# Later attention carried between the products of the layers

## The chip, the cores and the metric

One core of one Trainium2 chip runs the whole program. The metric is the device time of one execution in microseconds. The kernel before took 971.6 us (median of 3 runs, 970.73 to 973.06).

## What is computed

Three stages in a row, all in 32-bit floats:

```python
scores = scale * q @ k.T                    # 4 batches, 8 heads, 576 tokens, head width 64
scores = where(0 <= i - j < 128, scores - slope[h] * |i - j|, -1e9)
x = softmax(scores) @ v                     # then heads side by side: 2304 tokens x 512
x = (sigmoid(x @ w_gate) * (x @ w_val)) @ w_out      # hidden width 1536
out = ((x @ w1) * (x @ w2)) @ w3 @ w_out2            # hidden width 1024
```

## The kernel before

**Precision.** Each 32-bit operand is split into a high part (rounded to TensorE's fast 32-bit form) and a low part, the rest. A product is three matmuls: high x high, high x low, low x high (`product`, lines 424 to 426). The high part is a copy on ACT (sometimes DVE), the low part a subtraction on POOL or DVE.

**Attention.** A pair of heads of one batch is 5 steps of up to 128 queries, so 16 pairs are 80 steps. Step n passes through slots: scores (slot n + 4), masked and negated scores with their minimum on DVE (n + 5), exponentials on ACT, the row sums plus 1e-9 and their reciprocal on DVE, normalising on POOL (n + 6), four transposes on TensorE (n + 7), high and low part of the transposes, value product (n + 9), copy into `xf`. The queries of two heads stand as a block diagonal, so a scores matmul uses all 128 rows; a step is two blocks of 64 queries against 192 keys each. The program also multiplies `w3 @ w_out2` once (the fold): 64 products of 512 columns, one a slot, stored to memory. Attention has its own eight PSUM banks, laid under those of the layers.

**Layers.** The 2304 tokens go in three passes of 768, each in two halves of 384. A layer works in groups of 256 hidden columns (6 in the first, 4 in the second, where w3 is already in the folded output weights). Per group, `x @ w_gate` and `x @ w_val` (or w1, w2) are each a 2 x 2 block product done with seven block products and extra additions (`multiply`, `combine`); each block product is 6 matmuls of 384 columns. Sums of x (five tiles of its blocks, once per layer and pass) and sums of weights (once per group, on POOL in `weight_sum`) go in. Three banks hold the products, two the gates, three the output projection (`project`), which adds 8 tiles per group into `xf` (`add_up`). The projection of a group runs after the next group's products; the last one of a layer follows directly. Each engine's order is written out by hand, and engines meet by semaphores. Weights of group g + 1 are split while group g is multiplied (`weights_hi_plain`, `weights_hi_sums`, `weights_lo`). Where a layer begins, POOL also makes parts of the new x.

## Time and profile before

| | |
|---|---|
| profiled execution | 972.31 us, span 970.5 us |
| runs | 970.73, 971.6, 973.06 us |
| busy share | TensorE 93%, its weight loads 90%, DVE 71%, ACT 52%, POOL 74% |
| granted TensorE clock, mean | 0.979 |
| chain that ended last | TensorE 71%, DVE 14%, ACT 7%, issue 5%, POOL 2% |

The page shows one execution on the hardware profiler. PE is TensorE's matmuls, PEld its weight loads, SP the queue that issues the DMAs. A matmul's duration is its way through a pipeline: the next starts long before it ends, so throughput is read from starts. Idle time counts only on the engine that sets the end.

### The profile page before, as it was taken

To read this page: it belongs to the slowest core of one execution; us is meant where nothing else is said; L and a number is where in the kernel's file an instruction comes from. 1 tells how busy PE (TensorE), PEld (TensorE's weight loads), DVE (VectorE), ACT (ScalarE), POOL (GpSimd) and SP (SyncE) were. 2 spreads that over 40 slices of the span, in tenths; PEclk is the share of its full clock that TensorE was granted. 3 is DMA by queue.
4 is the path that set the end of the run, shared out by engine and by line. 5 is a ranking of instruction groups with operands and counts; after the bars stand their busy time and mean duration, and the time that the engine had idled before them with its cause. 6 is when DMAs were issued, how large, how long until landed. Compare 5 with 4: busy or idle time off the path is not lost.

```text
span 970.5 us, 15723 instructions
## 1 busy us (share of the span) xinstructions
PE 899.5 (93%) x5272; PEld 869.0 (90%) x5272; DVE 689.1 (71%) x1506; ACT 505.8 (52%) x1139; POOL 722.3 (74%) x535
## 2 busy tenths in 40 slices
PE   3999989868999997999999999799999999989998
PEld 3889877767899997899889999789988999988998
DVE  7988899885666668577756666857785666686666
ACT  4888878767544443544454444354444444435441
POOL 6778877876887775998679777489867977738940
PEclk9999999979999999999999999999999999998999
DMA  7333432410222210222142222012113211211301
GB/s 235 105 108 113 121 95 78 143 47 23 86 76 78 66 66 22 72 82 69 41 140 79 66 83 71 22 66 87 66 44 131 87 66 66 67 42 52 102 1 66
DMA packets 37409, 75.92 MB, mean 78 GB/s; under 512 B 3153, under 2 KB 16081, under 8 KB 37329
## 3 DMA queue, kind: packets, MB, share of 16 engines
q1 hardware_dynamic: 37328, 74.92, 23.9%
q8 instruction: 42, 0.69, 0.3%
q14 instruction: 39, 0.31, 0.1%
HBM read 68.09 MB, written 6.82 MB: 77 GB/s over the span
## 4 chain that ended last, share of the span: by engine, by line
PE 71%; DVE 14%; ACT 7%; issue 5%; POOL 2%; DMA 1%; SPq 0%; ACTq 0%; DVEq 0%; POOLq 0%
PE quad_ps L424 15%; PE quad_ps L426 14%; PE quad_ps L425 14%; PE o_ps L424 8%; PE o_ps L426 8%; PE o_ps L425 8%; DVE rowsum L766 3%; DVE xs_lo L811 2%; ACT exps L584 2%; DVE negs L755 1%; DVE xf L879 1%; POOL prob L1007 1%; ACT pt_hi L595 1%; DVE pt_lo L775 1%; ACT wq_hi L630 1%
## 5 line engine op out<-in xcount | busy, mean ns | idle before, releaser
L424 PE MATMUL quad_ps<-xs_hi,wq_hi 128*128 128x384 f32 x840 | 286.9, 342 | 25.4 <-ACT s L646 22.0
L426 PE MATMUL quad_ps<-xs_hi,wq_lo 128*128 128x384 f32 x840 | 284.6, 339 | 0.0
L425 PE MATMUL quad_ps<-xs_lo,wq_hi 128*128 128x384 f32 x840 | 284.5, 339 | 0.0
L424 PEld LDWEIGHTS quad_ps<-xs_hi,wq_hi 128*128 128x128 f32 x840 | 160.8, 191 | 31.7 <-issue 16.5
L1041 POOL TENSOR_TENSOR wq_lo<-wsum,wq_hi 128x1280 fp32r<-128x1280 f32 x60 | 177.3, 2955 | 9.4 <-ACT wq_hi L630 9.4
L424 PE MATMUL o_ps<-h_hi,wo_hi 128*128 128x384 f32 x480 | 161.2, 336 | 3.2 <-DVE xf L879 3.1
L425 PEld LDWEIGHTS quad_ps<-xs_lo,wq_hi 128*128 128x128 f32 x840 | 160.7, 191 | 0.0
L426 PEld LDWEIGHTS quad_ps<-xs_hi,wq_lo 128*128 128x128 f32 x840 | 160.5, 191 | 0.0
L426 PE MATMUL o_ps<-h_hi,wo_lo 128*128 128x384 f32 x480 | 160.4, 334 | 0.0
L425 PE MATMUL o_ps<-h_lo,wo_hi 128*128 128x384 f32 x480 | 160.4, 334 | 0.0
L1037 POOL TENSOR_TENSOR wq_lo<-raw_q,wq_hi 128x512 fp32r<-128x512 f32 x60 | 77.7, 1295 | 105.8 <-ACT wq_hi L624 105.8
L879 DVE TENSOR_TENSOR xf<-o_ps,xf 128x384 f32<-128x384 f32 x192 | 103.5, 551 | 43.6 <-PE o_ps L426 43.6
L661 ACT ACTIVATE gate_ps<-side 128x384 f32<-128x384 f32 x120 | 59.6, 498 | 76.4 <-DVE h_lo L867 55.4
L424 PEld LDWEIGHTS o_ps<-h_hi,wo_hi 128*128 128x128 f32 x480 | 90.1, 188 | 5.8 <-DVE xf L879 5.8
L646 ACT COPY s<-quad_ps 128x384 f32<-128x384 f32 x60 | 28.7, 479 | 120.2 <-PE quad_ps L426 120.1
L425 PEld LDWEIGHTS o_ps<-h_lo,wo_hi 128*128 128x128 f32 x480 | 90.1, 188 | 0.0
L426 PEld LDWEIGHTS o_ps<-h_hi,wo_lo 128*128 128x128 f32 x480 | 90.1, 188 | 0.0
L668 ACT CAST h_hi<-gate_ps 128x384 fp32r<-128x384 f32 x120 | 57.6, 480 | 59.6 <-DVE gate_ps L862 59.6
L1047 POOL TENSOR_TENSOR wo_lo<-raw_o,wo_hi 128x1024 fp32r<-128x1024 f32 x30 | 72.0, 2401 | 17.9 <-ACT wo_hi L638 17.9
L584 ACT ACTIVATE exps<-negs,negmax 128x192 f32<-128x192 f32 (+1 forms) x144 | 62.0, 432 | 42.9 <-DVE negmax L755 40.9
L867 DVE TENSOR_TENSOR h_lo<-gate_ps,h_hi 128x384 fp32r<-128x384 f32 x120 | 65.9, 549 | 23.8 <-ACT h_hi L668 23.3
L1062 POOL TENSOR_TENSOR wsum<-raw_q 128x512 f32<-128x512 f32 x60 | 81.8, 1363 | 0.0
(89 smaller groups left out, 1893.8 us busy)
## 6 DMA issues: line engine op xcount, KB each, us to landing
raw_q<-w SPq DMA_DIRECT2D x24, 512.0 KB, 3.5
raw_q<-w_gate SPq DMA_DIRECT2D x18, 512.0 KB, 3.5
raw_q<-w_val SPq DMA_DIRECT2D x18, 512.0 KB, 3.5
raw_o<-w_out SPq DMA_DIRECT2D x18, 512.0 KB, 3.5
raw_o<-w_times_wout SPq DMA_DIRECT2D x12, 512.0 KB, 3.6
k_raw<-kT SPq DMA_DIRECT2D x16, 288.0 KB, 2.9
q_raw<-qT SPq DMA_DIRECT2D x16, 288.0 KB, 3.0
v_raw<-v SPq DMA_DIRECT2D x16, 256.0 KB, 2.7
```

Source lines behind the costliest of these rows:

```text
L424: pe.matmul(out, lh, rh, start=start, stop=False, skip_group_check=onto)
L425: pe.matmul(out, lh, rl, start=False, stop=False, skip_group_check=onto)
L426: return pe.matmul(out, ll, rh, start=False, stop=stop, skip_group_check=onto)
L584: op = nc.scalar.activation(exps[buf][:, cols], negs[buf][:, cols], ACT.Exp, scale=-1.0, bias=negmax[:, 2 * buf + j:2 * buf + j + 1], accu ...
L661: nc.scalar.activation(gate_ps[n % 2][:, 0:TH], side[:, piece(k)], func).then_inc(gated, 1)
L668: nc.scalar.copy(h_hi[g % 2][:, piece(k)], gate_ps[n % 2][:, 0:TH]).then_inc(h_hi_done, 1)
L867: nc.vector.tensor_tensor(out=h_lo[g % 2][:, piece(k)], in0=gate_ps[n % 2][:, 0:TH], in1=h_hi[g % 2][:, piece(k)], op=ALU.subtract).then_i ...
L879: op = nc.vector.tensor_tensor(out=xf[:, cols], in0=ps_o[t % 3][:, 0:TH], in1=xf[:, cols], op=ALU.add)
L1037: nc.gpsimd.tensor_tensor(out=wq_lo[m][:, cols].rearrange("p (b n) -> p b n", b=2), in0=four[:, 0:4:3, :], in1=wq_hi[m][:, cols].rearrange ...
L1041: nc.gpsimd.tensor_tensor(out=wq_lo[m][:, 0:5 * GW], in0=wsum[m][:, :], in1=wq_hi[m][:, 0:5 * GW], op=ALU.subtract).then_inc(wq_split[m], 1)
L1047: nc.gpsimd.tensor_tensor(out=wo_lo[g % 2][:, :], in0=raw_o[:, :], in1=wo_hi[g % 2][:, :], op=ALU.subtract).then_inc(wo_split, 1)
L1062: op = nc.gpsimd.tensor_tensor(out=out[:, 2 * GW:4 * GW], in0=raw[:, 0:2 * GW], in1=raw[:, 2 * GW:4 * GW], op=ALU.subtract)
```

## The change

- **Attention is cut by thirds of the tokens.** The 80 steps are ordered by pass. The 28 of the first third (`HEAD`) run ahead of the layers, with two folds a slot. The other 52 are carried one per section inside the layers of pass one (24) and pass two (28).
- **Sections.** The layers' work is now a list of sections: gate (seven products), value (seven products), projection (eight tiles). A section issues the scores of step n first. The step of the section before has its transposes after the third product (or the third tile) and its value product after the sixth (or the seventh tile).
- **A step** is 128 queries of each of two heads against up to 256 keys. The scores are matmuls on 64 rows, heads alternating, each in its own bank. Softmax works in place in one tile. The addition of 1e-9 moves from DVE to ACT.
- **The block product** uses another formula with seven products and four sums of weights; products 1 and 2, and 7 and 4, accumulate in one bank. Results stay in four banks and the gate is kept in SBUF; no gate bank. The projection has two banks, attention two.
- **Tiles.** `xf` holds two thirds. Loaded raw tiles lie under the low parts that they become; the first loads wait for DVE's memsets. POOL makes four weight sums, a low part of three plain blocks and a low part of four sums.
- **x parts.** Of a layer's seven x blocks three are plain and four are sums; POOL makes one sum and four low parts (P1, P7, P3, P4), DVE the rest.

```diff
+PARTS = (((0, 0, 3), (0, 384, 2), (1, 0, 2)), ((1, 192, 3), (2, 0, 3)), ((2, 384, 2), (3, 0, 3), (3, 384, 2)))
+JOBS = [(third, hp, b, q0, n) for third in range(NPASS) for hp in range(HP) for b, q0, n in PARTS[third]]
+STEP = [(j, i) for j, job in enumerate(JOBS) for i in range(job[4])]
+FIRST = [STEP.index((j, 0)) for j in range(len(JOBS))]
...
+STEPS_TO = [sum(n for third, _, _, _, n in JOBS if third < t) for t in range(NPASS + 1)]
...
+P1, P5, P6, P2, P7, P3, P4 = range(7)
...
+A21, A11, A12, A22 = range(4)
...
+HALF_OF = {0: (C11, C12), 1: (C21, C22)}
+BANK_OF = {P1: 0, P2: 0, P6: 1, P3: 1, P5: 2, P7: 3, P4: 3}
+BANK_OUT = {C11: 0, C12: 1, C22: 2, C21: 3}
...
+LAG_QK, LAG_SCORE, LAG_NORM, LAG_TURN, LAG_PV = 3, 4, 5, 6, 8
+SLOTS = HEAD + LAG_PV
...
+def fold_slot(k):
+    return 5 + k // 2
+FOLDS_IN = [[k for k in range(NFOLD - IB) if fold_slot(k) == s] for s in range(SLOTS)]
...
+SECTIONS = []
+for g_ in range(NG):
+    SECTIONS += [(g_, "gate", g_), (g_, "val", g_)]
+    if not first_of(g_):
+        SECTIONS.append((g_, "proj", g_ - 1))
+    if last_of(g_):
+        SECTIONS.append((g_, "proj", g_))
...
+def step_at(sec):
+    t = sec // PASS_SECTIONS + 1
+    n = STEPS_TO[t] + sec % PASS_SECTIONS if sec >= 0 and t < NPASS else NSTEP
+    return n if t < NPASS and n < STEPS_TO[t + 1] else None
...
+        def twin(scope, name, shape):
+            with ExitStack() as first:
+                loaded = sb(first, f"{name}_raw", shape, F32)
+            return loaded, sb(scope, name, shape, F32R)
...
+        quad = [ps(f"quad_ps{k}") for k in range(4)]
+        ps_o = [ps(f"o_ps{k}") for k in range(2)]
+        attn = [ps(f"attn_ps{k}") for k in range(2)]
...
+            sp.wait_ge(zeroed, 1)
...
+                wait(pe, scored, n)
+                if n >= HEAD:
+                    drained = n in STEPS_TO
+                    pe.wait_ge(pt_split, n if drained else n - 1)
+                    pe.wait_ge(x_ready, n if drained else n - 1)
+                keys, q = keys_of(n), slice(i * P, (i + 1) * P)
+                first = JOBS[j][3] + (i - 1) * P - key_base(j)
+                where = slice(first + keys.start, first + keys.stop)
+                sides = ((q_hi, k_hi), (q_hi, k_lo), (q_lo, k_hi))
+                for t, (left, right) in enumerate(sides):
+                    for h in range(2):
+                        rows = slice(h * D, (h + 1) * D)
+                        mm = pe.matmul(score_bank(n, h)[:, keys], left[st][rows, q], right[st][rows, where],
+                                       start=t == 0, stop=t == 2)
                 mm.then_inc(qk_done, 1)
...
+            def consumed(q, blk):
+                if q % 2:
+                    pe.wait_ge(gated, 4 * (q // 2) + blk + 1)
+                else:
+                    wait(pe, h_split, 4 * (q // 2 - 1) + blk + 1)
...
+                if first_of(g) and m == 0:
+                    pe.wait_ge(xs_split[j], instance(g) + 1)
+                if j == P1:
+                    if q == 0:
+                        pe.wait_ge(scored, HEAD)
+                    else:
+                        consumed(q, C11)
+                elif j == P5:
+                    if q == 0:
+                        pe.wait_ge(pt_split, HEAD)
+                    else:
+                        consumed(q, C22)
+                elif j == P6 and q > 0:
+                    consumed(q, C12)
+                elif j == P7 and q > 0:
+                    consumed(q, C21)
+                elif j == P2:
+                    pe.wait_ge(s1_done, q + 1)
+                elif j == P3:
+                    pe.wait_ge(u2_done, q + 1)
+                elif j == P4:
+                    pe.wait_ge(c_done[C22], q + 1)
...
+                pe.wait_ge(h_split, 4 * g + 1 + max(HALF_OF[0][c], HALF_OF[1][c]))
+                wait(pe, acc_done, t - 1)
...
+            for k in range(NFOLD - IB, NFOLD):
+                fold(k)
+            for sec, (g, kind, of) in enumerate(SECTIONS):
+                n, m = step_at(sec), step_at(sec - 1)
+                if n is not None:
+                    scores(n)
+                if kind == "proj":
+                    for k in range(8):
+                        project(of, k)
+                        if k == 2 and m is not None:
+                            turn(m)
+                        if k == 6 and m is not None:
+                            pv(m)
                 else:
+                    for j in range(7):
+                        multiply(2 * g + (kind == "val"), j)
+                        if j == P6 and m is not None:
+                            turn(m)
+                        if j == P3 and m is not None:
+                            pv(m)
...
+                act.wait_ge(exp_done, n + 1)
+                wait(act, recip_done, n - 1)
+                nc.scalar.activation(rowsum2[0:rows, 2 * buf:2 * buf + 2], rowsum[0:rows, 2 * buf:2 * buf + 2],
+                                     ACT.Identity, bias=tiny[0:rows, 0:1]).then_inc(sum_done, 1)
...
+            for sec, (g, kind, of) in enumerate(SECTIONS):
+                n, m = step_at(sec), step_at(sec - 1)
+                more, inst = g + 1 < NG, instance(g) + 1
+                if kind == "gate":
+                    if g and first_of(g - 1):
+                        hidden_hi(g - 1, C21)
+                    keep(2 * g)
+                if kind == "val":
+                    gate(g, C21)
+                    keep(2 * g + 1)
+                if n is not None:
+                    exponentials(n)
+                if kind == "proj" and of == g - 1:
+                    hidden_hi(g, C21)
+                if m is not None:
+                    turned_hi(m)
+                splits(sec)
+                if kind == "gate":
+                    out_hi(g)
+                    gate(g, C11)
+                    if m is not None:
+                        out_copy(m)
+                    value_splits(sec)
+                    gate(g, C22)
+                    gate(g, C12)
+                elif kind == "val":
+                    if more:
+                        weights_hi(g + 1, 0)
+                    hidden_hi(g, C11)
+                    if m is not None:
+                        out_copy(m)
+                    value_splits(sec)
+                    hidden_hi(g, C22)
+                    hidden_hi(g, C12)
+                    if first_of(g):
+                        weights_hi(g + 1, 1)
...
+            def sums_26(q):
+                dve.wait_ge(prod_done, product_done(q, P6))
+                dve.wait_ge(s1_done, q + 1)
+                wait(dve, c_done[C21], q)
+                nc.vector.tensor_tensor(out=u2[:, :], in0=quad[1][:, 0:TH], in1=s1[:, :], op=ALU.add
+                                        ).then_inc(u2_done, 1)
+                dve.wait_ge(u2_done, q + 1)
+                wait(dve, c_done[C12], q)
+                nc.vector.tensor_tensor(out=u25[:, :], in0=quad[2][:, 0:TH], in1=u2[:, :], op=ALU.add
+                                        ).then_inc(u25_done, 1)
+            def result_22(q):
+                dve.wait_ge(prod_done, product_done(q, P7))
+                dve.wait_ge(u25_done, q + 1)
+                nc.vector.tensor_tensor(out=quad[2][:, 0:TH], in0=quad[3][:, 0:TH], in1=u25[:, :], op=ALU.add
+                                        ).then_inc(c_done[C22], 1)
+            def result_12(q):
+                dve.wait_ge(prod_done, product_done(q, P3))
+                nc.vector.tensor_tensor(out=quad[1][:, 0:TH], in0=quad[1][:, 0:TH], in1=u25[:, :], op=ALU.add
+                                        ).then_inc(c_done[C12], 1)
+            def result_21(q):
+                dve.wait_ge(prod_done, product_done(q, P4))
+                nc.vector.tensor_tensor(out=quad[3][:, 0:TH], in0=quad[3][:, 0:TH], in1=u2[:, :], op=ALU.add
+                                        ).then_inc(c_done[C21], 1)
...
+                if kind == "gate":
+                    if g and first_of(g - 1):
+                        hidden(g - 1, C21)
+                        hidden_lo(g - 1, C12)
+                        hidden_lo(g - 1, C21)
+                    sums_26(2 * g)
+                    if m is not None:
+                        turned_lo(m)
+                    if n is not None:
+                        reciprocals(n)
+                    result_22(2 * g)
+                    result_12(2 * g)
+                    result_21(2 * g)
+                elif kind == "val":
+                    sums_26(2 * g + 1)
+                    if m is not None:
+                        turned_lo(m)
+                    if n is not None:
+                        reciprocals(n)
+                    hidden(g, C11)
+                    result_22(2 * g + 1)
+                    hidden_lo(g, C11)
+                    hidden(g, C22)
+                    result_12(2 * g + 1)
+                    hidden(g, C12)
+                    hidden_lo(g, C22)
+                    result_21(2 * g + 1)
+                elif of == g - 1:
+                    add_up(of, 0)
+                    hidden(g, C21)
+                    add_up(of, 1)
+                    hidden_lo(g, C12)
+                    add_up(of, 2)
+                    hidden_lo(g, C21)
+                    if m is not None:
+                        turned_lo(m)
+                    if n is not None:
+                        reciprocals(n)
+                    for k in range(3, 8):
+                        add_up(of, k)
+                    if more and g % GP == GP - 1:
+                        x_sum(inst, P5)
...
+            def weight_sums(g, m):
+                def blk(b):
+                    return raw_q[m][:, b * GW:(b + 1) * GW]
+                def out(w):
+                    return wsum[m][:, (w - W_S1) * GW:(w - W_S1 + 1) * GW]
                 pool.wait_ge(rawq_in[m], 16 * (g + 1))
                 wait(pool, wq_split[m], g)
+                nc.gpsimd.tensor_tensor(out=out(W_S1), in0=blk(A21), in1=blk(A22), op=ALU.add
+                                        ).then_inc(wsum_done[m], 1)
+                nc.gpsimd.tensor_tensor(out=out(W_S3), in0=blk(A11), in1=blk(A21), op=ALU.subtract
+                                        ).then_inc(wsum_done[m], 1)
+                pool.wait_ge(wsum_done[m], 4 * g + 1)
+                nc.gpsimd.tensor_tensor(out=out(W_S2), in0=out(W_S1), in1=blk(A11), op=ALU.subtract
+                                        ).then_inc(wsum_done[m], 1)
+                pool.wait_ge(wsum_done[m], 4 * g + 3)
+                nc.gpsimd.tensor_tensor(out=out(W_S4), in0=blk(A12), in1=out(W_S2), op=ALU.subtract
+                                        ).then_inc(wsum_done[m], 1)
+            def plain_lo(g, m):
+                pool.wait_ge(wq_hi_done[m], 2 * g + 1)
+                nc.gpsimd.tensor_tensor(out=wq_lo[m][:, 0:PLAIN], in0=raw_q[m][:, GW:GW + PLAIN],
+                                        in1=wq_hi[m][:, 0:PLAIN], op=ALU.subtract).then_inc(wq_plain[m], 1)
+            def sums_lo(g, m):
+                pool.wait_ge(wq_hi_done[m], 2 * g + 2)
+                pool.wait_ge(wq_plain[m], g + 1)
+                nc.gpsimd.tensor_tensor(out=wq_lo[m][:, PLAIN:7 * GW], in0=wsum[m][:, :],
+                                        in1=wq_hi[m][:, PLAIN:7 * GW], op=ALU.subtract).then_inc(wq_split[m], 1)
...
+            for sec, (g, kind, of) in enumerate(SECTIONS):
+                n = step_at(sec)
+                more, inst = g + 1 < NG, instance(g) + 1
+                if kind == "gate":
+                    sums_lo(g, 1)
+                    if more:
+                        weight_sums(g + 1, 0)
+                elif kind == "val":
+                    out_lo(g)
+                    if more:
+                        weight_sums(g + 1, 1)
+                elif of == g - 1 and more:
+                    plain_lo(g + 1, 0)
+                    sums_lo(g + 1, 0)
+                if n is not None:
+                    normalise(n)
+                splits(sec)
+                if kind == "val" and first_of(g):
+                    plain_lo(g + 1, 0)
+                    sums_lo(g + 1, 0)
+                    plain_lo(g + 1, 1)
+                if kind == "proj" and of == g - 1 and more:
+                    plain_lo(g + 1, 1)
+                    if g % GP == GP - 1:
+                        x_lo(inst, P1)
+                if kind == "proj" and of == g and more:
+                    if g % GP == G1 - 1:
+                        x_lo(inst, P1)
+                    x_sum(inst)
...
```

## Rows read from the trace of the kernel before

**Rows 1.** The page's first part: busy us (share of span) x instructions.
```profile
PE 899.5 (93%) x5272; PEld 869.0 (90%) x5272; DVE 689.1 (71%) x1506; ACT 505.8 (52%) x1139; POOL 722.3 (74%) x535
```

**Rows 2.** Instructions by tile, folds and products: durations ns min/median/max, first and last start.
```profile
L424 PE MATMUL fold_ps<-wo_hi,w_hi x64: 473/477/776, 17.0 to 184.2; 128*128 128x512 f32 x64
...
L424 PE MATMUL quad_ps<-xs_hi,wq_hi x840: 334/334/689, 234.1 to 950.3; 128*128 128x384 f32 x168
```

**Rows 3.** TensorE in order of time, one slot: start us, us, instruction.
```profile
77.23 0.48 PE L424 MATMUL fold_ps<-wo_hi,w_hi 128*128 128x512 f32 x1
...
78.01 0.28 PE L424 MATMUL score_ps<-k_hi,q_hi 128*128 128x256 f32 x1
...
78.71 0.28 PE L424 MATMUL pv_ps<-pt_hi,v_hi 128*128 128x256 f32 x1
...
79.43 0.60 PE L455 MATMUL turn_ps<-eye,prob 128*128 128x128 f32 x4
79.78 0.48 PE L424 MATMUL fold_ps<-wo_hi,w_hi 128*128 128x512 f32 x1
```

**Rows 4.** Windows: stretch, length, busy PE, PEld, DVE, ACT, POOL, PEclk, DMA.
```profile
17.00:187.00 170.00, 157.15 (x1073) 138.94 (x1072) 150.31 (x498) 138.69 (x464) 133.28 (x146) 0.99 0.38 116
234.10:479.70 245.60, 235.53 (x1336) 231.78 (x1335) 167.69 (x299) 113.32 (x192) 190.92 (x118) 0.99 0.20 65
479.70:723.50 243.80, 233.62 (x1314) 230.45 (x1312) 166.00 (x297) 110.29 (x184) 189.36 (x116) 0.98 0.22 72
723.50:970.50 247.00, 235.73 (x1327) 233.49 (x1326) 157.84 (x294) 101.48 (x173) 161.01 (x100) 0.98 0.20 67
```

**Rows 5.** TensorE in order of time, layers: 18 matmuls apart, and the last.
```profile
300.02 0.33 PE L424 MATMUL quad_ps<-xs_hi,wq_hi 128*128 128x384 f32 x1
...
303.14 0.33 PE L424 MATMUL quad_ps<-xs_hi,wq_hi 128*128 128x384 f32 x1
...
967.28 0.34 PE L426 MATMUL o_ps<-h_hi,wo_lo 128*128 128x384 f32 x1
```

**Rows 6.** TensorE in order of time, second layer begins: [idle before <-releaser].
```profile
384.17 0.45 PE L424 MATMUL quad_ps<-xs_hi,wq_hi 128*128 128x384 f32 x1 [4.95 <-ACT s L646]
...
398.93 0.44 PE L424 MATMUL quad_ps<-xs_hi,wq_hi 128*128 128x384 f32 x1 [1.48 <-POOL wq_lo L1041]
```

**Rows 7.** The start in order of time: the first load's issue.
```profile
0.73 0.39 SPq L313 DMA_DIRECT2D k_raw<-kT  x1
```

**Rows 8.** DVE in order of time: the same instruction with POOL idle and POOL busy.
```profile
62.05 0.17 DVE L766 TENSOR_SCALAR rowsum<-rowsum 128x2 f32<-128x2 f32 x1
...
64.09 1.17 DVE L766 TENSOR_SCALAR rowsum<-rowsum 128x2 f32<-128x2 f32 x1
```

**Rows 9.** Groups by line, shapes apart: busy us, mean ns, idle before.
```profile
L1037 POOL TENSOR_TENSOR wq_lo<-raw_q,wq_hi 128x512 fp32r<-128x512 f32 x60 | 77.7, 1295 | 105.8 <-ACT wq_hi L624 105.8
...
L584 ACT ACTIVATE exps<-negs,negmax 128x192 f32<-128x192 f32 x112 | 50.3, 450 | 37.0 <-DVE negmax L755 36.3
...
L1007 POOL TENSOR_TENSOR prob<-exps,recip 128x384 f32<-128x384 f32 x48 | 41.5, 865 | 20.0 <-DVE recip L768 20.0
...
L755 DVE CUSTOM_DVE_ANT_0 negs<-score_ps,bias 128x192 f32<-128x192 f32 x112 | 34.9, 343 | 0.0
```

**Rows 10.** ACT in order of time: table load ahead of the first sigmoids.
```profile
240.19 1.28 ACT L661 ACT_TABLE_LOAD   x1
241.49 0.91 ACT L661 ACTIVATE gate_ps<-side 128x384 f32<-128x384 f32 x2
```

**Rows 11.** POOL in order of time, where the second layer begins.
```profile
377.64 2.54 POOL L1022 TENSOR_TENSOR xsum<-xf 128x768 f32<-128x768 f32 x1
...
385.24 2.00 POOL L1059 TENSOR_TENSOR wsum<-raw_q 128x512 f32<-128x512 f32 x1
...
388.44 0.75 POOL L1065 TENSOR_TENSOR wsum<-raw_q 128x256 f32<-128x256 f32 x1
389.13 2.40 POOL L1047 TENSOR_TENSOR wo_lo<-raw_o,wo_hi 128x1024 fp32r<-128x1024 f32 x1
...
395.93 2.94 POOL L1041 TENSOR_TENSOR wq_lo<-wsum,wq_hi 128x1280 fp32r<-128x1280 f32 x1
```

1384 lines of the change are left out of this document (651 added, 733 removed).

## Prediction

> **What bounds the kernel now.** I read the busy line first, then the windows by stage, then the matmuls in order of time, and last what stands before TensorE's gaps. TensorE is busy 93% of the span and no other engine over 74% [rows 1], but it is bound in two different ways. In the attention stage a slot comes each 2.65 us: 64 folds start from 17.0 to 184.2 us [rows 2]. Its matmuls need less: in a full slot the scores start 0.70 before the value product, that 0.72 before the transposes, those 0.35 before the fold, whose three matmuls take 0.78 [rows 3]. That is 1.87 for attention (with the 0.08 that the first fold after a transpose takes longer) and 0.70 for a fold. Two steps in five have half the transposes and half of one product, 1.29; the mean slot is 1.64 + 0.70 = 2.34. The missing 0.31 is the other engines' (DVE is busy 150 of 170 us) [rows 4]. In the layers, from 234.1 us on [rows 2], 18 matmuls of 384 columns start in 3.12 us, 0.1733 each [rows 5]. Both layers have (840 + 480) x 3 = 3960 of them, 686.3 us; from 234.1 to the last matmul at 967.3, plus its 0.17, are 733.4. So 47 us are lost there: the three windows show 10.1, 10.2 and 11.3 us of TensorE idle, and the rest is a granted clock of 0.98 to 0.99, that is stretches at 1.2 instead of 2.4 GHz [rows 4]. The longest gaps are where the second layer begins: 4.95, then 1.48 when POOL is late with the weights' low parts [rows 6]. The last matmul ends 3.1 us before the span does [rows 5].
>
> So the change must shorten the attention stage by more than what the same steps cost inside the layers. The sum by stages is 234.1 + 686.3 + 47 + 3.1 = 970.5.
>
> **The head.** 28 of the 80 steps stay ahead of the layers, with all the folding, now two folds a slot.
> - Start. Loads now wait until six memsets on DVE are done (the raw tiles share their place with the low parts); the first load was issued at 0.73 us [rows 7]. About 2.5 later; and eight low parts of wo2 fall in four slots instead of eight, about 1.5 more. First fold at 17.0 + 4 = 21.
> - 28 slots with two folds. Eight steps are short. Scores are now six matmuls on 64 rows, two heads side by side in two banks, 256 columns each as now. The trace has no 64-row matmul. Bounds: 0.35 (the two heads truly at once, half of 0.70) and 1.0 (nothing at once and a pipeline that must empty on both sides: a matmul lasts 0.33 and the next starts after 0.17, 0.16 each time [rows 5]). I take 0.70, today's. A full step is then 1.87, one that starts a batch (half the keys, one of two value products, two of four transposes) 0.98, the mean 1.62, with two folds 3.02. Over that I put 0.13 of waiting, under half of today's 0.31: the sum of 1e-9 leaves DVE for ACT, and that instruction took 0.17 us alone but 1.17 when POOL was in a long operation [rows 8]. DVE pays for it with 256 keys instead of 192 in the scores (0.34 becomes about 0.41, twice), ACT likewise (0.45 becomes 0.51), POOL's normalising goes from 384 to 512 columns, 0.87 to about 1.1 [rows 9]. All three stay under 3.15 a slot (ACT about 2.8). 28 x 3.15 = 88.
> - Three light slots, 6.3, and the last eight folds after them, 8 x 0.70 = 5.6. The x splits of the first products lie beside those folds.
> The head ends at 21 + 88 + 6.3 + 5.6 = 121. Bounds 112 (start at 19, slots 2.85) and 134 (slots 3.6).
>
> **Attention inside the layers.** 52 steps, 8 of them starting a batch (-0.89 each) and 8 with a block of 64 rows, 192 keys (-0.15): 52 x 1.87 - 8.3 = 89 us, bounds 71 and 105 by the scores' bounds. Nothing hides it, since TensorE is the bound. Products in the layers stay 3960 x 0.1733 = 686.3; another formula of seven products changes only the additions, which have slack.
>
> **Waits in the layers.** Worked out queue by queue. A gate or value section is now 7.3 + 1.9 = 9.2 us of TensorE, a projection section 10.1.
> - Four banks and no gate bank. The sums of products 1 and 6 must be read before product 3, with products 2 and 7 between (2.1 us for one addition on DVE); the next section's first use of a bank waits for a gate or a low part that ends about 1 us before. 0; below zero is excluded, for before has no wait there either.
> - New waits of TensorE at a section's head: scores(n) wait for the copy of the value product of step n - 2, and all products queue behind. The value product ends one product (1.04) before the section does, and ACT is then past the weights' high parts: 0, bounds 0 and 26 (0.5 a step). SP issues the loads of q, k and v between those of the weights, one job ahead; DMA is at 0.20 to 0.22 of its time there [rows 4]: 0.
> - Two instead of three banks for the projection. DVE comes to it late from the value section (it waits for ACT's hidden halves behind the weights' high parts). About 0.3 a group over 20 groups: 6; bounds 0 and 30 (1.5 a group).
> - ACT tables. Exponentials and sigmoids now alternate in the first layer of two passes: 2 x 6 x 2 = 24 more loads of 1.28 us [rows 10]. 31 us on ACT, which is busy 52%; what comes through is the value section's later hidden half, 0.3 a group: 4. Without cover 31.
> - POOL where the second layer begins. It does, after the last projection has begun, one sum of x and three low parts (four with the first) instead of two low parts and one sum. An operation on 768 columns took 2.54 there [rows 11]. Then it must pass seven sets before the second weights are ready. From 1024 columns in 2.40 and 1280 in 2.94 [rows 11] I get 2.1 ns a column and 0.25: 256 columns 0.8, 768 1.85. The queue is low part of sums 2.4, four sums 3.0 (started 0.05 inside each other), wo's low part 2.4, four sums 3.0, plain 1.85, sums 2.4: 15.0, where now it is 13.6 (385.24 to 398.87). The last low part of x ends about 17 us after the last projection began, and TensorE would be ready for the second group's weights at 8.3 + 14.6 = 23; they come at 32. 9 us each, with attention (its normalising and splits are as long as its matmuls) the same: 27 for three. Today's is 6.4.
> - POOL at the first layer's start: the same queue behind the x splits of the head, about 7. At the start of passes two and three x is ready early: 2.5 each, 5.
> - Clock. Of today's 47 us some 15 are lost at 1.2 GHz, in stretches that follow the long gaps. As many gaps remain, two of them shorter: 10.
> Together 6 + 4 + 27 + 7 + 5 + 10 = 59, against 47. Bounds 25 and 100.
>
> **The sum.** 121 + 686.3 + 89 + 59 + 3.1 = 958.4 of span, 12 under 970.5. The profiled execution's time is 972.3, 1.8 over its span and 0.7 over the median of 971.6: 958.4 + 1.8 - 0.7 = 959.5, about 960.
>
> **Two rules beside rows.** The load at 240.19 lasted 1.28 and the sigmoid started 1.30 after it began [rows 10]. The Trainium skill (ScalarE: Activation LUTs, "What ACT_TABLE_LOAD costs") puts a drain of about 1.38 us on top of each switch and advises to batch by set. By it the 24 loads would be 64 us of ACT and some 1.5 us more in each first-layer group: 18 us more, 978. The row shows no such drain, so I keep 1.28. On the 64-row scores, TensorEngine Tiling (Array Packing) in the Trainium skill, "Key Properties", says both that different tiles run in parallel and that a change of tiling mode drains TensorE; the one would take some 18 us off, the other add about as much. No row here shows either.
>
> **The rivals.**
> 1. POOL isn't late. If the first low parts come early enough and POOL runs ahead, the boundaries and the start cost 15 instead of 39, and the scores overlap a little (-8): 928. For it: POOL idles 106 us in 60 sets before its plain low part [rows 9]. Against: at the boundary TensorE waits for it already [rows 6]. 0.20.
> 2. The other side: POOL becomes the bound in the passes with attention. A pass of its own work is 10 x 17.4 + 28 x 1.1 + about 30 for q, k and v + 20 for x = 255 us, TensorE's 229 + 48 = 277. It decides from 8% more on POOL, when DVE's two-input operations hold it up, as in the 2.54 us rows [rows 11] against 1.85. If each section's chain (ACT high part, POOL low part, DVE reciprocal, POOL normalising, transposes) then runs late by 0.8, over 52 sections: 42 more, 999 in the worst; with half, 979. 0.20 at about 980.
> 3. The array empties around the 64-row scores and around the transposes between products: 0.16 three times a step in 80 steps is 38: 998. 0.08.
> 4. The table loads come through: they stand ahead of the gates and of the exponentials, on which DVE, POOL and the transposes hang. If 0.6 of 24 x 1.28 reaches TensorE, that is 18: 978. The drain that the Trainium skill adds would lead there. 0.05.
> 5. The change does in effect nothing: the head stays bound by DVE at 3.5 a slot (131) and the rest is as summed, 968 to 973. 0.07.
>
> **Chances.** The forecast (945 to 968) has 0.40, all of it faster. A difference of 0.2%, 2 us, is about what a measurement can tell from none. Faster: 0.40 + 0.20 + 0.03 = 0.63. Same: 0.05 (0.03 of rival 5, 0.02 of rival 2). Slower: 0.18 + 0.08 + 0.05 + 0.01 = 0.32. The range runs 928 to 990, which leaves out the ends of rivals 1, 2 and 3.
>
> **What would show it.** In the changed profile: the first product at 121 us (first fold at 21, 28 slots of 3.15); 0.70 from the first score matmul to what follows; 24 or so table loads of 1.28; at each second layer's start gaps before TensorE with POOL's low parts of the weights as their releaser, 9 us in sum; no long wait for normalising. I am wrong in the head if slots are over 3.4, in the layers if a steady gate section takes more than 9.4 us or a projection section over 10.6.

## The result, and the profile after

The changed kernel takes 1025.5 us (median of 4 runs, 1022.5 to 1028.0) where the kernel before takes 972.0 in the same comparison: a ratio of 1.055, interval 1.0516 to 1.0583. The forecast was 960, faster. The profiled execution spans 1022.5 us, 52.0 more than before.

Groups by tile of the changed kernel (durations ns min/median/max, first and last start), the answer to [rows 2]:

```profile
L576 PE MATMUL o_ps<-wo_hi,w_hi x64: 389/397/795, 17.8 to 131.5; 128*128 128x512 f32 x64
...
L576 PE MATMUL quad_ps<-xs_hi,wq_hi x840: 331/334/690, 132.8 to 1000.8; 128*128 128x384 f32 x168
```

The first fold starts at 17.8 and the first product at 132.8 (forecast 21 and 121), against 234.1 before. The windows answer to [rows 4], same columns (head, three passes):

```profile
17.00:133.00 116.00, 100.53 (x595) 75.93 (x596) 75.12 (x218) 75.92 (x256) 85.53 (x93) 0.99 0.35 111
132.80:440.00 307.20, 284.71 (x1686) 270.27 (x1684) 188.12 (x418) 181.21 (x393) 241.40 (x191) 0.96 0.22 73
440.00:767.00 327.00, 300.80 (x1757) 282.99 (x1756) 189.46 (x440) 191.00 (x443) 241.65 (x212) 0.95 0.22 73
767.00:1018.10 251.10, 236.64 (x1311) 232.18 (x1309) 145.17 (x265) 93.63 (x153) 162.83 (x124) 0.97 0.20 70
```

The third pass carries no step and takes 251 us, a little over the 247 of before. The first carries 24 steps and takes 307, the second 28 and 327. Take the length of a row less its first busy time: TensorE is idle 22 and 26 us in the passes with steps and 14 in the third, 63 in all, not some 10 each. And the clock, third from the end, is 0.96 and 0.95 in the first two, not 0.98 or 0.99. A mean of 0.96 over 307 us means 0.08 of them, 25 us, at 1.2 GHz; with 33 and 15 in the other passes that is some 72 us, where [rows 4] give 25.

What TensorE waited for in the changed kernel, its longest groups over the whole span (us in total, times, longest us):

```profile
PE quad_ps L576 <- POOL wq_lo L1290: 19.9, 5, 5.6
PE o_ps L576 <- DVE xf L1072: 12.3, 12, 3.8
PE o_ps L576 <- POOL w_lo L1325: 9.6, 7, 2.4
PE quad_ps L576 <- ACT sig L837: 9.3, 3, 5.2
PE attn_ps L614 <- DVE negmax L954: 8.8, 2, 6.0
```

In turn: the low parts of the weights on GpSimd, the additions of the projection on VectorE, the folds' low parts on GpSimd (in the head), the gates on ScalarE, and the transposes of carried steps, held until VectorE has done the next step's scores. One of each kind is followed below.

The carried scores in order of time (start us, us, instruction), the answer to [rows 3], where a group lasted 0.70:

```profile
301.76 0.34 PE L578 MATMUL o_ps<-h_hi,wo_lo 128*128 128x384 f32 x1
302.03 0.38 PE L599 MATMUL attn_ps<-k_hi,q_hi 64*128 64x256 f32 x2
302.25 0.28 PE L599 MATMUL attn_ps<-k_lo,q_hi 64*128 64x256 f32 x2
302.37 0.28 PE L599 MATMUL attn_ps<-k_hi,q_lo 64*128 64x256 f32 x2
302.58 0.44 PE L576 MATMUL o_ps<-h_hi,wo_hi 128*128 128x384 f32 x1
302.86 0.34 PE L577 MATMUL o_ps<-h_lo,wo_hi 128*128 128x384 f32 x1
```

Six matmuls of 64 rows stand in three pairs ("x2"), and the next matmul follows after 0.55: the two heads do run at once. But the changes of shape cost time on both sides: the first pair starts 0.27 after the product ahead of it, where products in the layers follow each other at 0.17, and the second pair 0.22 after the first, where the third follows at 0.12; behind the scores the starts are 0.21 and 0.28 apart.

ScalarE and SP's queue in order of time where the second pass begins:

```profile
439.99 0.39 SPq L501 DMA_DIRECT2D outT<-xf  x1
440.43 0.50 SPq L479 DMA_DIRECT2D raw_q<-w_gate  x1
440.97 1.01 SPq L488 DMA_DIRECT2D wo_lo_raw<-w_out  x1
```

```profile
449.12 1.04 ACT L818 CAST wo_hi<-wo_lo_raw 128x1024 fp32r<-128x1024 f32 x1 [5.29 <-DMA wo_lo_raw<-w_out]
450.18 1.28 ACT L837 ACT_TABLE_LOAD   x1
451.47 0.49 ACT L837 ACTIVATE sig<-quad_ps 128x384 f32<-128x384 f32 x1
```

```profile
452.11 0.66 PE L576 MATMUL quad_ps<-xs_hi,wq_hi 128*128 128x384 f32 x1 [3.34 <-ACT sig L837]
```

The store of the finished pass waits for its last addition, and both loads of the new pass stand behind it. ScalarE copies the output weights ahead of the first gate, so that the gate, and TensorE for 3.34 us, wait for a load that had no reason to be late. At the third pass it is 7.98 and 5.22. The table load lasted 1.28 and the sigmoid began 1.29 after it did, as in [rows 10]; there are 25 of them.

Section by section, the steady part is as forecast. From one section's first product to the next one's, a gate or value section of the first pass mostly takes 9.2 us and a projection section 10.1, the forecast's own figures; the second pass has medians of 10.4, 9.2 and 10.6. The long ones stand where a layer begins: up to 18.6 for a gate section.

Where the span's 52.0 us are, with two of the experiments below as steps between (first and last matmul of the layers read in each trace):

```
head, to the first product            234.1 -> 132.8      -101.3
layers without any carried step       733.4 -> 766.4       +33.0   (before -> e1)
TensorE's own instructions of 52 steps  766.4 -> 843.1     +76.7   (e1 -> e2)
the steps' work on the other engines  843.1 -> 885.5       +42.4   (e2 -> changed)
after the last matmul                   3.1 -> 4.3          +1.2
```

### The profile page after: what moved, and what is told of

It is laid out like the page before. It is cut to its first block, busy times and chain, and to the rows that moved or that the text cites. A ratio compares the mean times of both kernels' runs of the same rounds, so it can differ in the third digit from the quotient of the medians.

```text
span 1022.5 us, 16149 instructions
## 1 busy us (share of the span) xinstructions
PE 924.7 (90%) x5352; PEld 862.7 (84%) x5352; DVE 605.3 (59%) x1364; ACT 548.9 (54%) x1259; POOL 736.3 (72%) x626
## 4 chain that ended last, share of the span: by engine, by line
PE 69%; POOL 14%; DVE 6%; issue 4%; ACT 3%; DMA 2%; SPq 1%; DVEq 0%; ACTq 0%; POOLq 0%
PE quad_ps L576 12%; PE quad_ps L577 11%; PE quad_ps L578 11%; PE o_ps L576 9%; PE o_ps L578 8%; PE o_ps L577 8%; POOL wq_lo L1290 3%; PE attn_ps L599 2%; PE attn_ps L576 2%; PE attn_ps L614 2%; POOL xs_lo L1254 2%; DMA wo_lo_raw<-w_out 2%; POOL wq_lo L1283 1%; POOL soft L1239 1%; DVE xf L1072 1%
## 5 line engine op out<-in xcount | busy, mean ns | idle before, releaser
L576 PE MATMUL quad_ps<-xs_hi,wq_hi 128*128 128x384 f32 x840 | 298.9, 356 | 37.7 <-POOL wq_lo L1290 19.9
L576 PE MATMUL o_ps<-h_hi,wo_hi 128*128 128x384 f32 x480 | 168.7, 351 | 12.8 <-DVE xf L1072 12.3
L1290 POOL TENSOR_TENSOR wq_lo<-wsum,wq_hi 128x1024 fp32r<-128x1024 f32 x60 | 143.4, 2390 | 7.7
L1021 DVE TENSOR_TENSOR u<-quad_ps,s 128x384 f32<-128x384 f32 x60 | 33.4, 557 | 179.4 <-PE quad_ps L578 176.3
L1283 POOL TENSOR_TENSOR wq_lo<-raw_q,wq_hi 128x768 fp32r<-128x768 f32 x60 | 110.5, 1841 | 36.8 <-ACT wq_hi L810 36.8
L1239 POOL TENSOR_TENSOR soft<-soft,recip 128x512 f32<-128x512 f32 (+2 forms) x80 | 73.3, 917 | 77.0 <-DVE recip L965 76.8
L771 ACT ACTIVATE soft<-soft,negmax 128x256 f32<-128x256 f32 (+2 forms) x160 | 75.0, 470 | 50.8 <-DVE negmax L954 50.6
L843 ACT CAST h_hi<-quad_ps 128x384 fp32r<-128x384 f32 x120 | 56.0, 478 | 63.9 <-DVE quad_ps L1055 63.5
L1296 POOL TENSOR_TENSOR wo_lo<-wo_lo_raw,wo_hi 128x1024 fp32r<-128x1024 f32 x30 | 71.8, 2392 | 20.7 <-ACT wo_hi L818 20.7
L794 ACT COPY xf<-attn_ps 64x128 f32<-64x128 f32 (+1 forms) x160 | 39.3, 246 | 75.3 <-PE attn_ps L578 74.2
```

Of the source, the lines that this page charges most:

```text
L576: pe.matmul(out, lh, rh, start=start, stop=False, skip_group_check=onto)
L771: op = nc.scalar.activation(cols, cols, ACT.Exp, scale=-1.0, bias=negmax[0:rows, 2 * buf + h:2 * buf + h + 1], accum_out=rowsum[0:rows, 2 ...
L794: op = nc.scalar.copy(out_cols(n, h), pv_bank(n)[h * D:(h + 1) * D, h * P:h * P + rows])
L843: nc.scalar.copy(h_hi[g % 2][:, piece(blk)], quad[BANK_OUT[blk]][:, 0:TH]).then_inc(h_hi_done, 1)
L1021: nc.vector.tensor_tensor(out=u2[:, :], in0=quad[1][:, 0:TH], in1=s1[:, :], op=ALU.add).then_inc(u2_done, 1)
L1239: nc.gpsimd.tensor_tensor(out=cols, in0=cols, in1=recip[0:rows, 2 * buf:2 * buf + 2].unsqueeze(2).to_broadcast([rows, 2, keys.stop - keys. ...
```

## The experiments

All times are medians of runs beside runs of the kernel before (971.5 to 972.3). "Late store" is e3; each later one says what it stands on.

A run's time holds the head too, and most edits leave the head alone. So here is each trace by stage, in us: the first product, and the layers from there to the last matmul.

| | first product | layers |
|---|---|---|
| changed kernel | 132.8 | 885.4 |
| e3 late store | 136.9 | 872.7 |
| e4 | 137.6 | 882.8 |
| e5 | 133.8 | 879.5 |
| e6 | 132.7 | 872.0 |
| e7 | 132.3 | 868.5 |
| e8 | 122.8 | 873.3 |
| e9 | 123.8 | 867.4 |
| e10 | 123.3 | 857.7 |
| e11 | 125.5 | 857.8 |
| e12 | 123.0 | 854.3 |
| e13 | 123.2 | 838.6 |

The head of the changed kernel and of e3 to e7 is the same, yet it ends anywhere from 132.3 to 137.6. The mean granted clock from 17 to 132 us is 0.99 where it ends early and 0.93 in e3 and e4. The trace of e3, on which e5 to e8 stand, has a long head, so a difference of times to it may hold up to 4.6 us that no edit made.

**e1, no carried steps.** Their loads, scores, softmax, transposes and value products are left out, so the layers work on zeros there.

```
 def step_at(sec):
+    return None
```

> Left out: the attention of the second and third thirds (52 steps: loads, scores, softmax, transposes, value products); the layers then work on zeros there. What stays is the head of 28 steps and the layers with seven products in four banks and two output banks. Theory (carried steps cost, banks do not): first product near 132 us, layers as long as before's 736.4 plus the 7 us at the start, about 877 to 885 us in all, so the 52 steps cost about 140 us, 2.7 each. Rival (the four banks or the two output banks cost time by themselves, a few us a section): above 905 us.

Measured 903.8 us, ratio 0.9307 (0.9289 to 0.9326). It falls between the two, nearer the rival: the 52 steps cost 121.7, 2.34 each, and not 140; the layers by themselves lost 33 us against before. Its waits name them: the gate behind the store 11.4 us, GpSimd's weights 11.1 (before 3.2), the additions 8.4 (3.1); waits for ScalarE's copy of the first product fell from 22.0 to 10.4. In all TensorE is idle 20 us more; most of the rest is clock.

**e2, TensorE's instructions of the steps alone.** The other engines do nothing of the 52 steps; TensorE runs the same shapes on old tiles.

> Left out: everything of the 52 carried steps except TensorE's own instructions (12 score products, 2 or 4 transposes, 3 or 6 value products a step, same shapes and places, on tiles left over from the head), so nothing on the other engines and no load. Theory A (TensorE's instructions, with the switches between 64-row and 128-row products, are about half of the cost): 73.8 us of spacing plus 10 to 20 us of switches over the first kernel of this call, so 960 to 975 us. Rival B (the instructions are nearly all of it): 1005 us or more. Rival C (the clock makes up for them; nearly all of the cost is waits): 935 to 950 us.

Measured 979.7 us, ratio 1.009 (1.0072 to 1.0109): 75.9 us over e1, 1.46 a step. This is a little above theory A. A step has six matmuls for the scores (not the twelve that I wrote above). The steps' matmuls follow each other at 0.06 (scores, two at once), 0.11 (transposes) and 0.12 (value products), 73.8 us in all; the changes between them and the products cost some 0.36 a step, 18.6 us; shorter waits and less time at 1.2 GHz gave back 16 of it, since TensorE arrives later at what was late. 73.8 + 18.6 = 92 is the forecast's 89. The remaining 45.8 us of the changed kernel come from the other engines' part of the steps.

**e3, late store.**

```
-                    if g and g % GP == 0:
-                        store_pass(g // GP - 1)
                     if g + 1 < NG:
                         load_quad(g + 1, 0)
                     load_out(g)
+                    if g and g % GP == 0:
+                        store_pass(g // GP - 1)
```

> The store of a finished pass is issued behind the loads of its gate section, not ahead of them. Theory: the output weights of the new pass's first group come some 10 us earlier, ACT's copy of them no longer waits (5.29 and 7.98 us) and the 3.34 and 5.22 us that TensorE waits for the gates go, with some of the low clock behind them: 8 to 13 us faster than the changed kernel, 1013 to 1018 us. Rival: what is late next (GpSimd's low parts of the weights, DVE's x work) ends at the same place: 0 to 4 us, 1021 to 1025 us.

Measured 1014.5 us, ratio 1.0436 (1.0401 to 1.0472): 11 us, the theory; the layers of its trace are 12.7 shorter. ScalarE's wait for these weights, first of the changed kernel and then here:

```profile
ACT wo_hi L818 <- DMA wo_lo_raw<-w_out: 22.7, 7, 8.0
```

```profile
ACT wo_hi L818 <- DMA wo_lo_raw<-w_out: 13.4, 6, 2.5
```

**e4, no sigmoid.** The first layer's gate is a plain copy; 24 table loads go.

```
-                func = ACT.Sigmoid if g % GP < G1 else ACT.Copy
+                func = ACT.Copy
```

> Left out: the sigmoid of the first layer; its gate is a plain copy, so the 24 table loads of 1.28 us in the layers go and nothing else changes. Theory (the forecast's 4 us for them): 2 to 7 us faster than the changed kernel, 1018 to 1023 us. Rival (ACT stands 1.28 us later at each switch and the products wait for it, 24 x 1.28 = 31 us): below 1000 us.

Measured 1022.3 us, ratio 1.053 (1.0502 to 1.0559), 3 us less, which the intervals don't tell from none. Most of the 24 x 1.28 = 31 us of ScalarE stay beside other work; the forecast's 4 fits, and its rival 4 (18) falls.

**e5, four sections of the first pass without a step** (on e3).

```
+SKIP = {1: (0, 1, 18, 19), 2: ()}
```

> On top of the late store: the 24 steps carried in the first pass leave out four sections, the first two of the pass and the first two of its second layer (28 steps in the second pass fill all sections that they may use, so that pass is unchanged). Theory (a carried step in the sections where VectorE's x sums and GpSimd's weights are already late costs more than elsewhere): the 5.99 us before the transposes at the second layer's start, about 3 us of GpSimd's low parts behind it and 2 to 4 us at the pass start go, 8 to 13 us faster than the late store alone (1014.5), 1002 to 1007 us. Rival (the work only moves; the same sum of work on GpSimd and VectorE is late elsewhere): 0 to 3 us.

Measured 1016.3 us, ratio 1.0459 (1.0443 to 1.0475): no gain, the rival. By its trace the layers are even 7 us longer. The 6.00 us before the transposes went. TensorE in the changed kernel, then here:

```profile
324.56 1.09 PE L614 MATMUL attn_ps<-eye,soft 128*128 128x128 f32 x4 [6.00 <-DVE negmax L954]
```

```profile
324.00 0.66 PE L585 MATMUL quad_ps<-xs_hi,wq_hi 128*128 128x384 f32 x1 [3.16 <-ACT s L833]
```

so the layer's start is slow with or without the step.

**e6, four banks for the last projection section of a pass** (on e3).

```
+            return (ps_o + attn)[t % 4] if t // 8 % GP == GP - 1 else ps_o[t % 2]
```

> On top of the late store: the eight output tiles of each pass's last projection section go round four banks (the two output banks and the two attention banks, which are free there). Theory (two banks let TensorE stop whenever VectorE puts a 2 us x sum between two additions): the waits for the additions of 12.3 us fall by half, with some clock, 5 to 9 us faster than the late store alone (1014.5). Rival (VectorE is the bound over the whole stretch, so that the next product waits for its x parts instead): 0 to 2 us.

Measured 1009.3 us, ratio 1.0383 (1.0366 to 1.0400): 5 us, by the time the edge of the theory. By stage it is the rival: the layers are 0.7 us shorter, and the other 4.2 lie in the head, which the edit leaves alone. The waits for additions fell from 12.3 to 4.7, those for GpSimd's weights rose from 20.6 to 24.5, and one wait came back at the section's end, where the next scores need the same banks:

```profile
437.46 0.58 PE L605 MATMUL attn_ps<-k_hi,q_hi 64*128 64x256 f32 x2 [5.25 <-DVE xf L1083]
```

**e7, the carried steps' normalising on ScalarE** (on e3).

```
+                    op = nc.scalar.activation(cols, cols, ACT.Copy,
+                                              scale=recip[0:rows, 2 * buf + h:2 * buf + h + 1])
```

> On top of the late store: the normalising of the 52 carried steps is done by ScalarE (two activations with the reciprocal as scale) and not by GpSimd. Theory (GpSimd is what is late in the layers: 20.6 us of waits for its low parts of the weights): these waits fall by a third to a half, 6 to 12 us faster than the late store alone (1014.5). Rival (ScalarE, later by two instructions of some 0.4 us a step, becomes late for the gates and the copies): no faster or up to 10 us slower.

Measured 1006.8 us, ratio 1.0369 (1.0345 to 1.0394): 8 us, the theory in time, but not by its way: the waits for GpSimd's weights fell only from 20.6 to 17.4, those before the transposes from 8.8 to 5.7, and TensorE waits 4.7 us for ScalarE's output copies instead. Of the 8.9 us between the two traces 4.6 lie in the head; the layers gain 4.2, below the theory, and more of it by less time at 1.2 GHz than by shorter waits.

**e8, all low parts of w3 on VectorE** (on e3).

```
-                if s in W3_LO_SLOT and W3_LO_SLOT[s] % 2:
+                if s in W3_LO_SLOT:
```

> On top of the late store: the eight halves of the fold's low parts that GpSimd makes (1.27 us each) are made by VectorE (1.08 us each) as the other eight are. Theory (GpSimd sets the head's slots: folds wait 8.6 to 9.6 us for its low parts): first product 5 to 9 us earlier (132.8 to 137.6 now), the layers unchanged, 1006 to 1010 us. Rival (the softmax chain over VectorE is as long): first product at most 2 us earlier or later, 1013 to 1018 us.

Measured 1001.4 us, ratio 1.0317 (1.0291 to 1.0343): 13 us, more than the theory, and all of it in the head (layers 873.3 against 872.7). Its first product:

```profile
L575 PE MATMUL quad_ps<-xs_hi,wq_hi x840: 333/334/690, 122.8 to 978.5; 128*128 128x384 f32 x168
```

122.8 against 136.9 in the late store's trace and 132.8 in the changed kernel's, so 10 us are the edit's and the rest is the late store's long head. No fold waits for a low part any more. Three of the ten come ahead of the slots: the first fold starts at 14.8, not 17.8.

**e9, e10, e11.** e9 is e3, e6, e7 and e8 together. e10 adds the later low part of a layer's first output weights; e11 the new order of the x parts.

```
                 elif kind == "val":
-                    out_lo(g)
+                    if not first_of(g):
+                        out_lo(g)
```

> The late store, the four output banks, the normalising on ScalarE and the fold's low parts on VectorE together. Theory (four separate places, so that the gains of 11, 5, 8 and 13 us under the changed kernel's 1025.5 add up): 986 to 991 us. Rival (one releases what another held, so that they overlap): 993 to 1000 us.

> The same, and the low part of the output weights of each layer's first group (2.4 us of GpSimd, six times), which stands in front of the next group's weights though its projection comes four sections later, is moved behind them by a section. Theory (GpSimd's queue is what the products at the start of each layer's second group wait for, 1.6 to 5.3 us): 1.6 to 2.4 us at each of six places, 9 to 14 us under the combined kernel. Rival (it is late there by another piece, ScalarE's high parts): under 4 us.

> The same, and the x parts at each layer's start in another order: ScalarE makes the high parts that need no sum first and keeps the first product ahead of the last two of them, GpSimd takes the first x part before the keys and queries, VectorE takes the last x sum after the step's scores, and at a pass's end the first sum goes into the section before. Theory (the order on the three engines and not their load makes the 6.0 us before the transposes and the 3.4 us before the fourth product at a second layer's start): 4 to 6 us at each of three second layers and 1 to 2 at each of two pass starts, 14 to 20 us under the kernel before it in this call, so about 960 to 968 us, below the kernel before the change. Rival (load: the same parts are late again by their sum): 0 to 5 us.

Measured 996.8, 988.6 and 988.0 us (ratios 1.0252, 1.0185, 1.0169, each 0.002 to 0.003 either way). e9's time is the rival's, but the traces show no overlap: from the changed kernel's layers take e3's 12.7, e6's 0.7 and e7's 4.2, and 867.8 are left, where e9 has 867.4. The sum in the theory was too large because three of its four differences counted the late store's long head as a gain. The move of six instructions of 2.4 us gives 8 (just under the theory; 9.7 in the layers); the new order gives nothing (the rival). At the second layers' starts e10 still had waits of 2.8 before the transposes and, in the last pass, 3.45 before the fourth product (the 6.0 was already gone). The new order left no more than 1.3 of any of them and made another of 5.25, for keys that GpSimd now splits behind three x parts, a low part and four weight sums. Its trace also shows why two engines' shares do not add. VectorE and GpSimd in order of time:

```profile
602.83 0.96 DVE L1045 TENSOR_TENSOR xt<-xf,xt 128x768 f32<-128x768 f32 x1
603.71 2.60 DVE L1051 TENSOR_TENSOR xs_lo<-xt,xs_hi 128x768 fp32r<-128x768 f32 x1
```

```profile
602.88 2.61 POOL L1288 TENSOR_TENSOR xt<-xf 128x768 f32<-128x768 f32 x1 [1.82 <-DVE xf L1110]
605.45 2.56 POOL L1294 TENSOR_TENSOR xs_lo<-xf,xs_hi 128x768 fp32r<-128x768 f32 x1
```

A two-input operation of 768 columns from memory takes VectorE 0.94 and GpSimd 1.82 where the other engine is idle; in these four lines the first on VectorE takes its own time, and each one that starts while the other engine is at work lasts about 2.6, nearly the two together. The Trainium skill (SBUF — State Buffer, "Who interferes with whom") calls the port pair that these two engines share an exclusive lock and says that a VectorE instruction with two inputs in SBUF contends with a GpSimd instruction that reads SBUF; the durations agree.

**e12, less on GpSimd** (on e11). VectorE makes most low parts of the output weights and one more of x, and GpSimd splits keys and queries ahead of the weight sums.

```
+                    if g and not last_of(g - 1):
+                        out_lo(g - 1)
```

> On top of the kernel with the new order (988.0): the low parts of the output weights go from GpSimd (2.4 us each) to VectorE for all groups but each layer's last, the last x part's low half too, GpSimd makes the keys' and queries' low parts ahead of the weight sums, and at a second layer's start VectorE adds the last two output tiles before it makes low parts. Read before: a 128x768 subtraction from memory to memory takes VectorE 0.95 us when GpSimd rests and 2.1 to 2.6 us beside one of GpSimd's, which then takes 2.5 and not 1.84. Theory (the two engines share a path to memory, so work that moves to VectorE costs half as much of it): the waits for GpSimd's weights of 19.4 us halve, 10 to 18 us faster, 970 to 978 us. Rival (VectorE, 62% busy, becomes late for the sums of the products): 985 us or more.

Measured 982.8 us, ratio 1.0118 (1.0097 to 1.0140): 5 us, between the two. VectorE took 1.38 in the mean for what took GpSimd 2.4. Both sides show. VectorE did become late for the sums of the products, as the rival had it, a wait that e11 does not have:

```profile
PE quad_ps L579 <- DVE quad_ps L1079: 7.3, 5, 2.7
```

And the new order in GpSimd's queue made one gap longer than any before. GpSimd, then TensorE:

```profile
630.85 0.73 POOL L1279 TENSOR_TENSOR v_lo<-v_lo_raw,v_hi 128x256 fp32r<-128x256 f32 x1 [7.66 <-ACT v_hi L774]
```

```profile
639.13 0.69 PE L579 MATMUL quad_ps<-xs_hi,wq_hi 128*128 128x384 f32 x1 [8.00 <-POOL wq_lo L1343]
```

The values' low part waits 7.66 us for ScalarE, with four weight sums and two low parts queued behind it that need nothing of ScalarE's late work. The changed kernel had the pattern already: at 656.81 this low part waits 2.59 us for ScalarE, and TensorE 5.16 for the weights behind it.

**e13 and e14, the queues** (on e12). What may wait goes last in GpSimd's section; a step's output copy goes ahead of the next one's normalising on ScalarE; VectorE makes the last x part's low half behind a sum of products, not ahead of it; e14 adds the scores one product later.

```
                 splits(sec)
                 if kind == "val" and first_of(g):
                     plain_lo(g + 1, 0)
                     sums_lo(g + 1, 0)
+                value_splits(sec)
```

> On top of the last kernel (982.8): GpSimd's order in each section, so that nothing that waits for ScalarE stands ahead of the weight sums and of a next group's low parts (there its v_lo waited 7.66 us for ScalarE and TensorE then 8.15 us for GpSimd; 5.12 and 2.98 at two other places); ScalarE copies a step's output ahead of its normalising; VectorE makes the last x part's low half behind the product sum and not ahead of it. Theory (what is left of the loss is the order in the queues): 8 to 12 us for the three places and 4 to 6 for the scores that waited for the copy, 965 to 972 us, at or below the kernel before the change. Rival (these places are late by their load): 978 to 983 us.

> The same with a step's scores behind the first product or output tile of its section, not ahead of it. Theory (scores at the head of a section wait up to 1 us for the copy of an earlier step's output or for keys, which one product covers): 2 to 6 us under the kernel before it in this call. Rival (the chain over VectorE and the transposes is then late by the same microsecond): 0 to 5 us slower.

Measured 967.4 us for e13, ratio 0.9953 (0.9939 to 0.9967), below the kernel before; 969.7 for e14, ratio 0.9986 (0.9973 to 1.0000), so the later scores cost 2 (the rival). e13 is the theory in full, 15 us. Its windows, then its three longest groups of waits in the layers:

```profile
123.20:431.00 307.80, 290.36 (x1749) 274.18 (x1748) 205.68 (x442) 207.88 (x459) 212.09 (x166) 0.99 0.26 85
431.00:745.00 314.00, 298.55 (x1805) 280.11 (x1803) 208.21 (x458) 215.53 (x501) 214.03 (x181) 1.00 0.24 78
745.00:961.60 216.60, 210.96 (x1198) 207.37 (x1197) 143.26 (x253) 81.34 (x134) 129.16 (x99) 1.00 0.18 60
```

```profile
PE o_ps L579 <- DVE xf L1119: 11.9, 14, 1.7
PE quad_ps L579 <- POOL wq_lo L1343: 7.9, 6, 2.6
PE quad_ps L579 <- DVE xs_lo L1054: 6.2, 7, 2.2
```

TensorE's waits for VectorE's sums of products are gone. No wait in the layers is over 2.6 us, and the clock is at 2.4 GHz nearly throughout (0.99, 1.00, 1.00).

## Why the prediction was wrong

**Right.** The kind of sum, and several terms. TensorE's share of the carried steps was 89 us and is 92 by its spacings (e2), and a steady section takes the forecast's 9.2 and 10.1. The 0.70 for the scores was luck: they run at once, which takes 0.35 off, and the changes of shape give it back. Table loads: 25 of 1.28, about 3 us of time and not clear of noise (e4). 7 at the first layer's start is 5.6 and 0.8.

**Right in size only.** The gaps at the three second layers' starts, forecast at 9 each, are 10.2, 11.4 and 8.4 by adding the gaps over 0.4 us there. The forecast's cause was POOL's low parts of the weights, and of these gaps only 3.0, 5.2 and 3.0 are theirs; the others wait for VectorE (scores, x parts), for keys, or for ScalarE's copy.

**The head, 121 against 132.8.** The step that failed is "0.13 of waiting" a slot. Slots come every 3.79 us, not 3.15 (and over 3.4, the forecast's own sign of being wrong): GpSimd's half of w3's low parts stands in the queue of the normalising, and about every fourth slot the folds wait for it. I priced each engine's work per slot (all under 3.15) and not the one long instruction that comes in some of the slots. e8 takes it out; its slots still come every 3.52, and that it lands at 122.8, near the forecast, is luck in part: its first fold starts at 14.8, where 21 was forecast (17.8 in the changed kernel). From the first fold to the first product are 115 us in the changed kernel, 108 in e8 and 100 in the forecast, so 7 of 15 are this instruction, and the other 8 stay open.

**The layers, "Together 59" against 107.** (885.5 less 686.3 and 92.) The forecast had 49 of waits and 10 of clock. The changed kernel has 63 of idle TensorE and about 26 of clock; the remaining 18 or so are matmuls that start a little over 0.1733 apart without a gap, and no run looks into them. Three of the terms failed:
- "SP issues the loads ...: 0" and "at the start of passes two and three x is ready early: 2.5 each". I read only the loads of q, k and v in SP's queue and not the store of the finished pass, which stands ahead of the new pass's weights. With VectorE's x sums between the additions the two pass starts lose about 11 and 10 us (the waits for additions of the next point among them). The store alone is 11 us of time (e3).
- "Two instead of three banks: 6". The waits for additions are 12.3 us, in the pass's last sections. But four banks in their place gain 0.7 us in the layers (e6), so the number of banks is not what costs there.
- "Clock: as many gaps remain: 10". Of the 72 us at 1.2 GHz TensorE lost about 26 by comparing its spacing there with 0.1733. In the layers' trace a stretch at 1.2 GHz stands behind every wait of 3 us and more, and behind some of 1.9 to 3.0. Over the 63 us of idle that is about 0.4 us more for each us of gap, which was priced at its own length. In e13, with no wait over 2.6, the loss is under 2.

Three smaller slips of the forecast. Its rows give 1.85 and not 1.87 for attention in a slot. The third window's 11.3 of idle holds the 3 us behind the last matmul. And [rows 4] give some 25 us at 1.2 GHz, which can lose at most half of that, 12, and not "some 15": the rest of before's 47 was slow spacing too.

**How far the order of the queues was the cause.** The rival of the other side, GpSimd held up by VectorE, had a mechanism that is there (2.6 us instructions side by side) and nearly the size. But load is not all: e12 and e13 have the same work on each engine (GpSimd 545 and 556 us in the layers, VectorE 558 and 557) and differ by 15 us. From the changed kernel to e13 the layers get 46.8 us shorter, by the table 12.7 by the late store, some 10 by e10's move, 15.7 by e13's order, and GpSimd's busy time falls by 13% (736.3 to 637.8 us), part of it in the head. e13's layers, with every step in them, are 4.5 us shorter than e2's, where the other engines do nothing of the steps. So waits that one queue passes to the next are a large part of what the carrying seemed to cost. How large a part of the 45.8 is not shown: the fixes also act on the 33 us that the layers lose without steps (e1), and no run takes the steps out of e13. With the fixes the kernel takes 967.4, against the forecast of 960 and 972 before.

What stays open: the 38 us of idle TensorE left in e13's layers are by their waits 14 for VectorE's additions, 8 for GpSimd's weights, 6 for x parts, and the rest in small ones; no run took any of these out alone. I also gave the change's side effects in the layers without steps (e1: 33 us) no place of their own; the store, the additions and GpSimd's order are named by e1's waits, but only the first two were tried singly, and that with the steps in place.

## What to carry to other kernels

When work is threaded into a full pipeline, TensorE's price is the easy term; read each queue in program order at every stage boundary, SP's too, and ask of each instruction that may wait what stands behind it that does not need it. A long instruction in some slots is not its mean over all slots. Price a gap of several us with the slow stretch behind it. And when an edit touches one stage, compare that stage in the traces: here 4 to 5 us of three gains lay in a stage that the edit left alone.

## What the runs showed of the hardware

- Matmuls of 64 rows on the two halves of the array do run at once: pairs of 256 columns start together and the next pair 0.12 later. Going from products of 128 rows to such pairs costs about 0.2 in all, and going back about 0.2 (starts of 0.27 and 0.22 where 0.17 and 0.12 are usual, then 0.21 and 0.28 where 0.12 and 0.17 are). The Trainium skill (TensorEngine Tiling (Array Packing), "Key Properties") states that different tiles run in parallel and that a change of tiling mode drains TensorE; the two nearly cancel here.
- VectorE and GpSimd on two-input operations of 768 columns from memory: 0.94 and 1.82 alone, 2.6 and 2.6 together. For 1024 columns VectorE took 1.38 in the mean and GpSimd 2.4, so from e11 to e12 GpSimd's busy time in the layers fell by 54 us and VectorE's rose by 38.
- Waits of 1 to 2.6 us left the granted clock in e13's layers at 2.4 GHz but for one stretch of 3.4 us (0.99 to 1.00); the changed kernel, with waits of 3 to 6, had 0.95 to 0.97. No safe length follows: in the changed kernel stretches at 1.2 GHz also stand behind waits of 1.9 and 3.0 us.
